# Row maximum of a score tile: bank 0 by itself, banks 1 and 2 in one instruction

## The reference

```
q_pool = q.reshape(B, H, S // 2, 2, D).mean(axis=3)        # B=2, H=8, S=1152, D=64
scores = (1/8) * matmul(q_pool, k.T)                       # 576 x 1152 for each b, h
scores = scores - max(scores, axis=-1)
attn   = exp(scores); attn = attn / (sum(attn) + 1e-9)
x      = matmul(attn, v)                                   # then rows of 512
x      = moe(x)      # two products, width 2048, a rational function between them
out    = moe2(x)     # gate, value and output products, width 1536, after an RMS norm
```

## Time and profile before

| | before |
|---|---|
| median of 3 runs | 690.28 us (687.85 to 690.89) |
| profiled execution, device time | 688.53 us |
| its span in the profile | 686.7 us |
| TensorE matmul busy | 670.4 us, 98% |
| VectorE busy | 514.0 us, 75% |
| ScalarE busy | 411.0 us, 60% |
| GpSimd busy | 443.7 us, 65% |

### The profile page before, as it was taken

How to read it: one execution, slowest core, us unless ns; L and a number is a source line. 1 busy time by engine, 2 the same in 40 slices (tenths; PEclk the granted TensorE clock), 3 DMA queues, 4 the chain that set the end, 5 groups by cost and what they waited for, 6 DMA issues and landing times.

```text
span 686.7 us, 11834 instructions
## 1 busy us (share of the span) xinstructions
PE 670.4 (98%) x3940; PEld 622.1 (91%) x3940; DVE 514.0 (75%) x1005; ACT 411.0 (60%) x860; POOL 443.7 (65%) x440
## 2 busy tenths in 40 slices
PE   7899999999999999989999999999999999999998
PEld 5899999999999999879999999899999999999996
DVE  6899999999999958987899889977544444444432
ACT  5778878887887778987888888844511111111110
POOL 5887999998999979998789789854624440000000
PEclk9999999999999999999999999999999999999999
DMA  8567468666645420210110110123111200000012
GB/s 234 183 169 205 123 174 244 174 181 163 193 153 142 101 88 0 62 61 2 62 62 0 63 63 1 62 71 115 61 63 47 77 0 1 1 0 1 1 61 77
DMA packets 26012, 60.76 MB, mean 88 GB/s; under 512 B 3304, under 2 KB 7920, under 8 KB 25840
## 3 DMA queue, kind: packets, MB, share of 16 engines
q1 hardware_dynamic: 25680, 59.87, 29.6%
q10 hardware_dynamic: 288, 0.33, 0.2%
HBM read 43.78 MB, written 2.40 MB: 67 GB/s over the span
## 4 chain that ended last, share of the span: by engine, by line
PE 82%; DVE 5%; POOL 4%; ACT 3%; issue 2%; DMA 2%; SPq 0%; DVEq 0%; POOLq 0%; ACTq 0%
PE hb L906 28%; PE ob L963 21%; PE sc L808 11%; PE sc L816 9%; PE misc L834 5%; PE pv_ps L834 5%; PE tb L906 3%; DVE neg_part L1205 1%; POOL num L767 1%; DMA km_lo<-kqB 1%; POOL num L765 1%; DMA qrawA<-in_q 1%; DMA o_part<-o_sb 1%; DVE num L1265 1%; ACT num L1101 1%
## 5 line engine op out<-in xcount | busy, mean ns | idle before, releaser
L1036 ACT ACTIVATE pt_hi<-sc 128x384 fp32r<-128x384 f32 x216 | 90.5, 492 | 46.7 <-PE sc L816 46.7
L1205 DVE TENSOR_REDUCE neg_part<-sc 128x1 f32<-128x384 f32 x216 | 107.4, 549 | 11.5 <-PE sc L808 10.5
L1214 DVE TENSOR_TENSOR pt_lo<-sc,pt_hi 128x384 fp32r<-128x384 f32 x216 | 106.5, 549 | 2.6 <-ACT pt_hi L1036 1.5
L963 PE MATMUL ob<-wo_hi,gt_hi 128*128 128x512 f32 x252 | 99.6, 395 | 3.9 <-DVE tok L1290 3.9
L963 PE MATMUL ob<-wo_lo,gt_hi 128*128 128x512 f32 x252 | 99.1, 393 | 0.0
L963 PE MATMUL ob<-wo_hi,gt_lo 128*128 128x512 f32 x252 | 99.0, 393 | 0.0
L906 PE MATMUL hb<-xt_hi,wi_hi 128*128 128x384 f32 x280 | 94.6, 338 | 0.6 <-DVE xt_lo L1246 0.4
L906 PE MATMUL hb<-xt_lo,wi_hi 128*128 128x384 f32 x280 | 94.1, 336 | 0.0
L906 PE MATMUL hb<-xt_hi,wi_lo 128*128 128x384 f32 x280 | 94.0, 336 | 0.0
L1027 ACT ACTIVATE prob<-sc,neg_max 128x1152 f32<-128x1152 f32 x72 | 89.1, 1238 | 2.5 <-DVE neg_max L1207 2.5
L816 PE MATMUL sc<-ident,prob 128*128 128x128 f32 x648 | 83.1, 273 | 1.4 <-ACT prob L1027 1.4
(11 more groups left out here) (172 smaller groups left out, 1702.3 us busy)
## 6 DMA issues: line engine op xcount, KB each, us to landing
wraw<-in_moe_w_out SPq DMA_DIRECT2D x6, 1024.0 KB, 5.2
krawB<-in_k SPq DMA_DIRECT2D x8, 576.0 KB, 4.4
qrawB<-in_q SPq DMA_DIRECT2D x8, 512.0 KB, 5.9
krawA<-in_k SPq DMA_DIRECT2D x7, 576.0 KB, 4.3
o_part<-o_sb SPq DMA_DIRECT2D x14, 288.0 KB, 4.1
qrawA<-in_q SPq DMA_DIRECT2D x7, 512.0 KB, 5.3
wraw<-in_moe_w_in SPq DMA_DIRECT2D x3, 1024.0 KB, 5.2
wraw<-in_moe_w_gate SPq DMA_DIRECT2D x3, 1024.0 KB, 5.2
```

Source lines behind the costliest of these rows:

```text
L963: ins = nc.tensor.matmul(ob[(m + 1) % 2][:], gt[i][:, f, P * t:P * t + P], wo[c % 2][j][:, f, :], start=f == 0 and n == 0, stop=f == CHUNK ...
L1036: nc.scalar.activation(pt[0][:, 3 * c:3 * c + 3, PT_COL[i]:PT_COL[i] + P], src, ACT.Copy).then_inc(pt_hi, 1)
L1205: nc.vector.tensor_reduce(neg_part[:, s, c:c + 1], sc[s][:, c, 0:KBANK], AX.X, ALU.max, negate=True).then_inc(part_done, 1)
L1214: nc.vector.tensor_tensor(pt[1][:, kt, col], src, pt[0][:, kt, col].bitcast(F32), ALU.subtract).then_inc(pt_lo, 1)
```

## The change

The reductions of banks 1 and 2 become one instruction, over both inner dimensions (`AX.XY`) of a 128x2x384 view. It waits for all three banks. `neg_part` has two columns instead of three. The last wait of `row_max` counts two signals for each tile instead of three. The other engines' instructions and waits stay as they were.

```diff
-        neg_part = sbuf(top, "neg_part", [P, 2, 3])
+        neg_part = sbuf(top, "neg_part", [P, 2, 2])
...
             def row_max(i, h, s):
                 n = (h * 9 + i) * 3
-                for c in range(3):
-                    dve.wait_ge(qk_done, n + (c + 1))
-                    nc.vector.tensor_reduce(neg_part[:, s, c:c + 1], sc[s][:, c, 0:KBANK], AX.X, ALU.max, negate=True).then_inc(part_done, 1)
-                dve.wait_ge(part_done, n + 3)
+                dve.wait_ge(qk_done, n + 1)
+                nc.vector.tensor_reduce(neg_part[:, s, 0:1], sc[s][:, 0, 0:KBANK], AX.X, ALU.max, negate=True).then_inc(part_done, 1)
+                dve.wait_ge(qk_done, n + 3)
+                nc.vector.tensor_reduce(neg_part[:, s, 1:2], sc[s][:, 1:3, 0:KBANK], AX.XY, ALU.max, negate=True).then_inc(part_done, 1)
+                dve.wait_ge(part_done, (h * 9 + i) * 2 + 2)
                 nc.vector.tensor_reduce(neg_max[:, s:s + 1], neg_part[:, s], AX.X, ALU.min).then_inc(max_done, 1)
```

## The result

The kernel got slower. Before and after ran six times each in this comparison: medians 689.20 us (687.85 to 690.89) and 694.73 us (693.67 to 695.38). The ratio is 1.0076, 95% interval 1.0059 to 1.0092, which is a loss of 4.1 to 6.3 us. The forecast was +0.76% or 5.2 us. The profiled execution of the kernel after took 694.37 us, with a span of 692.5 us.

The account below looks back on a forecast made before the run. TensorE sets the pace, with VectorE close behind; joining adds a loop through bank 2. Seven heads x 0.72 = 5.0 us plus 0.2 in head 0 gave 5.2 us, +0.76%: 693.7, or 695.4 on the median's footing; range 691.5 to 699.

Parts of the forecast that it names:

- The bound and the place: Attention: TensorE sets the pace with VectorE close behind; short 3.11 us tiles lengthen, long 3.38 us ones hide the wait.
- the loop: From pt_lo through bank 2's load, scores, joined and small reductions back to pt_lo: 3.24 us, above 3.11, below 3.38.
- The joined instruction: VectorE's reduction of 768 elements takes 0.95 us, bounds 0.78 and 1.10; occupied time shrinks 0.07 us for each tile.
- The walk through the head: Head 6 as example: TensorE gets 0.12, 0.25, 0.42, 0.62, then 0.72 us late; tiles 5 to 8 add nothing.
- Head 0: First three tiles run into the 2.03 us DMA wait for km and cost nothing; 0.2 us counted after it.
- Behind the attention: The stages behind the attention move as they are, with nothing added.
- Held loads: TensorE's weight loads waiting for pt_lo go up from 15 places to about 35, five in a head.
- step 3: pt_lo of tile 2 starts at 195.23 instead of 194.81; TensorE already waits for its first bank, so 0.42 us late.
- The dearer reduction: Rival: the joined reduction costs 1.10 us, so even long tiles don't hide it; 699.5 or 701 us; chance 0.12.
- No change: Rival: at 0.78 us the loop is 3.07, below 3.11, and nothing is left; 690.3 us; chance 0.20.
- faster: Rival: VectorE already over 0.25 us late, so only 0.07 us for each tile counts; 685.3 or 687.8 us; chance 0.06.
- The rule of the Trainium skill: A large tile pays a fixed latency once, many small ones each time; by it alone the kernel gets faster.

Follow-up runs that it names:

- joined_1to5: Kernel before with the joined reduction only in tiles 1 to 5 of each head, three reductions in the others; 695.34 us, ratio 1.0082.
- joined_0and6to8: Kernel before with the joined reduction only in tiles 0, 6, 7 and 8 of each head; 688.83 us, ratio 0.9992.
- three_wait: Kernel before, three reductions kept and nothing joined, but that of bank 1 also waits for bank 2; 697.69 us, ratio 1.0122.
- all_joined: Against the kernel after: all three banks in one reduction that gives the maximum itself, small reduction gone; 705.86 us, ratio 1.0224 to the kernel before.
- joined_lo_first: Kernel after with pt_lo of bank 0 put ahead of the small reduction in VectorE's queue; 690.22 us, ratio 1.0011 to the kernel before.
- banks01_joined: Against the kernel after: banks 0 and 1 joined, bank 2 reduced by itself; 696.54 us, ratio 1.0099 to the kernel before.
- before_again: The kernel before, unchanged, run once more for a second profile; 688.96 us, one run.

## Why the prediction was right

**The time.** The mechanism held, and the size too, but that both percentages read 0.76 is luck: the interval of the measured ratio is 2.3 us wide. In absolute time the forecast on the profile's footing, 693.7 us, met 694.37, and the one on the median's, 695.4, met 694.73. The second rests on a median of three runs, 690.28, and six runs of the same kernel gave 689.20. Between the two profiles lie 5.8 us: 5.07 in heads 1 to 7 and 1.3 behind the attention, less 0.55 in head 0. Of these the first was forecast, as 5.0, and for head 0 0.2 more.

**The bound and the place.** Right. joined_1to5 has all of the loss and joined_0and6to8 none. From the transposes of tile 0 to those of tile 5 in head 6, the kernel before takes 3.11, 3.11, 3.39 (the mixed tile's scores), 3.05 and 3.15 us, and the one after 3.25, 3.25, 3.54, 3.25 and 3.26. These five leave no room beside the loop. The long periods of 3.38 do, and they stayed as they were, 3.37 us from the small reduction at 188.29 to that at 191.66 in the profile after.

**The joined instruction.** Taken as 0.95 us, measured 0.957. The bounds of 0.78 and 1.10 were far off.

**The added wait and the loop.** Added up to 3.24 us, measured 3.25. The same sum gave 3.31 for three_wait (measured 3.31), 3.47 for all_joined (3.45) and 3.14 for joined_lo_first (3.13). banks01_joined was the weakest, 3.25 against 3.29. That is one sum five times, each time with another term changed, and it is the best evidence for the loop. The sums of the experiments were made when the 0.96 and the 3.25 us of the change were known, so what they test is which terms change, and the first sum alone was made from the profile before.

**The walk through the head.** It said TensorE would be 0.12, 0.25, 0.42, 0.62 and 0.72 us late. The transposes of tiles 1 and 2 are 0.14 and 0.28 late. For tiles 3 to 5 these are the rows of before (the last one was cut by the end of the view, two transposes short):

```profile
197.11 1.14 PE L816 MATMUL sc<-ident,prob 128*128 128x128 f32 x9
200.16 1.19 PE L816 MATMUL sc<-ident,prob 128*128 128x128 f32 x9
203.31 0.93 PE L816 MATMUL sc<-ident,prob 128*128 128x128 f32 x7
```

After, they start at 200.51, 203.76 and 207.02. Less the 2.97 of tile 0 that is 0.43, 0.63 and 0.74. For all of heads 1 to 7 the small reductions give the sum. First and last of the kernel before:

```profile
38.73 0.16 DVE L1207 TENSOR_REDUCE neg_max<-neg_part 128x1 f32<-128x3 f32 x1
240.59 0.16 DVE L1207 TENSOR_REDUCE neg_max<-neg_part 128x1 f32<-128x3 f32 x1
```

and after:

```profile
38.18 0.15 DVE L1208 TENSOR_REDUCE neg_max<-neg_part 128x1 f32<-128x2 f32 x1
245.11 0.15 DVE L1208 TENSOR_REDUCE neg_max<-neg_part 128x1 f32<-128x2 f32 x1
```

That is 201.86 and 206.93 us, 5.07 more, where seven times 0.72 gave 5.0. In before_again the same stretch took 201.54 us, so by that profile it is 5.39: two profiles of one kernel differ by 0.3 us here.

**Head 0.** I counted 0.2 us and said that the first three tiles cost nothing behind the wait for `km`. This can't be checked, and the second half was too simple. In the profile after, head 0 is 0.55 us shorter (38.73 to 38.18), and its mixed tile started earlier, because the keys were there and it waited for `pt_lo` instead:

```profile
18.75 0.41 PE L808 MATMUL sc<-km_hi,qm 128*128 128x384 f32 x1 [0.81 <-DVE pt_lo L1215]
```

In joined_1to5 the same matmul starts at 20.62 after 2.78 us of waiting for the DMA, in banks01_joined at 21.65. This landing scatters by some 3 us from run to run, so it hides 0.2 us completely. When it is early, the change can cost something in head 0 too; no run shows how much.

**Behind the attention.** "The stages behind move as they are" holds for the change but not for the two profiles. Before, 686.7 - 240.59 = 446.1 us follow the last small reduction, after, 692.5 - 245.11 = 447.4. The 1.3 us are the stretch at the lower clock. In before_again, 687.2 - 239.91 = 447.3 us follow, too, and in joined_0and6to8, the other profile without such a stretch, 687.9 - 241.88 = 446.0. Against before_again the change costs 692.5 - 687.2 = 5.3 us, all of it in heads 1 to 7.

**Held loads.** I said about 35, five in a head, and there are 41, up to six in a head. Bank 1 is held in step 3 as well (the load at 202.84), which the walk left out. Bank 2 waits right behind it, so it adds nothing to the time.

**The rivals.** The dearer reduction fell to the 0.957. "No change" and "faster" needed a shorter instruction or a VectorE that is already 0.25 us late. It is idle in front of 56 of the 72 joined ones, 0.24 us in the short periods. The rule of the Trainium skill ("VectorE: DVE Perf Modes", section on the TRN2 errata), that a large tile pays a fixed cost once, points the right way for the instruction alone, though that section speaks of instructions that read SBUF, and these reductions read PSUM. The joined one occupies 0.88 us (banks01_joined, 78.04 to 78.92) against 0.94 for two, and three_wait against the change shows those 0.06 us in the period. Joining also moves its start back to its last input, and that cost more than it gave.

## What to carry to other kernels

Before joining two instructions that consume the pieces of a producer one by one, see whether the consumer has caught up with the producer. If it has, the joined instruction waits with work in hand, and everything behind it in the queue is late by that much. Add up the loop that runs through the last piece and compare it with the pace of the engine that sets the end, tile by tile: here the same edit was free beside 3.37 us and cost 0.14 beside 3.11. Where such a loop bounds, look for idle time of the queue inside it, such as a small dependent instruction that waits for its input, and put ready work there.

## What the runs showed of the hardware

A maximum over 384, 768 and 1152 float32 elements of one, two and three banks takes 0.549, 0.957 and 1.358 us. The two steps of 384 elements and one bank add 0.408 and 0.401 us, 1.06 and 1.04 ns for each element. The earlier trace rows have 1.05 ns for each element between two-operand instructions of 384 and 512 elements, so little can be left for the crossing into another bank. No run here has the crossing without the elements.

TensorE's granted clock was at its lower level, 1.2 of 2.4 GHz, in a stretch of the feed-forward stage, after a wait of 2.5 to 2.8 us for VectorE. In the profile after, where it was 0.50 of full speed from 303 to 305 us:

```profile
302.04 0.74 PE L963 MATMUL ob<-wo_hi,gt_hi 128*128 128x512 f32 x1 [2.77 <-DVE tok L1291]
302.58 0.63 PE L963 MATMUL ob<-wo_hi,gt_lo 128*128 128x512 f32 x1
...
305.56 0.40 PE L963 MATMUL ob<-wo_lo,gt_hi 128*128 128x512 f32 x1
```

The matmuls take 0.63 us for 3.5 us and then 0.40 again. before_again had the same after a wait of 2.49 us, and the first profile before had none after one of 2.51 us. Of the ten profiles eight have it, after waits of 2.49 to 2.83 us, and two have none, after 2.49 and 2.51 us. Much the same wait is thus followed by the lower clock in one run and not in another. Head 0 shows it once more, after the wait for `km`: the clock was at 0.50 from 22 to 24 us in joined_1to5 and in banks01_joined, after waits of 2.78 and 3.78 us, and stayed up in joined_lo_first after one of 3.02 us. What decides it stays open. In the feed-forward stage it costs about 1.2 us (447.3 against 446.1 us behind the attention, for one and the same kernel). So two single profiles can differ by that much without any change, and more when head 0 has it too.
